# High and low value halves in one stationary for four of nine key blocks, the missing column summed by GpSimd; key copy by DMA; first expert weights split in pieces

## The reference, cut to what matters

```python
q_pool = q.reshape(B, H, S // 2, 2, D).mean(axis=3)          # [2, 8, 576, 64]
scores = scale * np.matmul(q_pool, k.transpose(0, 1, 3, 2))  # [2, 8, 576, 1152]
attn = np.exp(scores - np.max(scores, axis=-1, keepdims=True))
attn = attn / (np.sum(attn, axis=-1, keepdims=True) + 1e-09)
x = np.matmul(attn, v)                                        # [2, 8, 576, 64] -> 1152 tokens x 512
# then a mixture of 8 experts with the top two for each token (512 -> 1024 -> 512, relu),
# then h = x @ w_in [512, 2048];  out = (h * cos(h)) @ w_out
```

## Time and profile before

| | us |
|---|---|
| median of 3 runs | 854.96 |
| profiled execution: time | 854.54 |
| profiled execution: span of its instructions | 852.8 |
| TensorE matmuls busy | 838.9 |
| TensorE weight loads busy | 744.4 |
| VectorE busy | 499.0 |
| ScalarE busy | 422.2 |
| GpSimd busy | 402.5 |

### The profile page before, as it was taken

One profiled execution on the slowest core, in us unless ns is written; L12 is line 12 of the kernel. 1 busy time (PEld: TensorE's weight loads), 2 busy tenths in 40 slices (PEclk: granted clock), 3 DMA queues, 4 the chain that ended last, 5 costly groups with the idle time before them and its releaser, 6 DMA issues.

```text
span 852.8 us, 15404 instructions
## 1 busy us (share of the span) xinstructions
PE 838.9 (98%) x4868; PEld 744.4 (87%) x4869; DVE 499.0 (59%) x995; ACT 422.2 (50%) x776; POOL 402.5 (47%) x293
## 2 busy tenths in 40 slices
PE   7999999999999999999999999999999999999998
PEld 6899999999999888888887888888888888999997
DVE  7788877888877887322232222222276776676664
ACT  3777777777777763212111211111145665564554
POOL 8554445555877104648959959577532030000000
PEclk9999999999999999999999999999999999999999
DMA  5112211142232015987645545363444020000101
GB/s 146 53 43 62 64 42 42 42 142 67 92 130 102 1 56 181 310 298 241 237 151 172 197 148 184 118 214 115 155 133 152 1 75 27 12 1 0 38 1 38
DMA packets 51521, 91.28 MB, mean 107 GB/s; under 512 B 9376, under 2 KB 18592, under 8 KB 50976
## 3 DMA queue, kind: packets, MB, share of 16 engines
q1 hardware_dynamic: 40832, 67.26, 23.5%
q0 software_dynamic: 3360, 11.01, 4.4%
q10 hardware_dynamic: 7296, 12.59, 4.4%
HBM read 73.78 MB, written 17.06 MB: 107 GB/s over the span
## 4 chain that ended last, share of the span: by engine, by line
PE 89%; DVE 5%; ACT 2%; issue 2%; POOL 2%; DMA 0%; DVEq 0%; POOLq 0%; ACTq 0%
PE ps L1640 10%; PE ps L1642 10%; PE ps L1641 10%; PE ps L1460 5%; PE ps L1490 5%; PE ps L1506 4%; PE ps L1508 4%; PE ps L1507 4%; PE ps L1491 4%; PE ps L1766 4%; PE ps L1767 4%; PE ps L1765 4%; PE ps L1752 3%; PE ps L1750 3%; PE ps L1751 3%; PE ps L1679 2%
## 5 line engine op out<-in xcount | busy, mean ns | idle before, releaser
L639 POOL TENSOR_TENSOR W<-stage,W 128x2048 fp32r<-128x2048 f32 x32 | 147.3, 4602 | 2.6
L1023 DVE TENSOR_REDUCE mx<-ps 128x1 f32<-128x384 f32 x225 | 119.6, 551 | 17.8 <-PE ps L1460 17.8
L1035 DVE TENSOR_TENSOR pl__80<-ps,ph 128x576 fp32r<-128x576 f32 x144 | 108.0, 750 | 33.5 <-ACT ps L793 33.4
L788 ACT ACTIVATE ph<-ps 128x576 fp32r<-128x576 f32 x144 | 93.9, 652 | 53.5 <-PE ps L1491 52.4
L793 ACT ACTIVATE ps<-ps 128x576 f32<-128x576 f32 x144 | 93.5, 649 | 0.0
L1506 PE MATMUL ps<-ph,vs 128*65 128x288 f32 x288 | 86.1, 299 | 0.4 <-ACT ot L747 0.4
L862 ACT CAST hh<-ps 128x512 fp32r<-128x512 f32 x50 | 26.9, 590 | 119.2 <-PE ps L1679 115.2
L1490 PE MATMUL ps<-qat,kt 128*128 128x288 f32 x288 | 83.8, 306 | 1.3 <-ACT qbt L740 0.6
L1508 PE MATMUL ps<-ph,vs 128*65 128x288 f32 x288 | 84.8, 294 | 0.0
L1507 PE MATMUL ps<-pl__80,vs 128*65 128x288 f32 x288 | 84.6, 294 | 0.0
L1640 PE MATMUL ps<-W,xh 128*128 (+1 forms) x200 | 80.4, 402 | 1.3 <-POOL W L639 0.7
(11 more groups left out here) (220 smaller groups left out, 1960.8 us busy)
## 6 DMA issues: line engine op xcount, KB each, us to landing
stage<-in_moe_w_dram SPq DMA_DIRECT2D x32, 1024.0 KB
y_slots<-ys ACTq DMA_DIRECT2D x25, 256.0 KB
x_slots<-ring SPq DMA_DIRECT2D x22, 256.0 KB
xs<-x_slots ACTq DMA_DIRECT2D x22, 256.0 KB
kn<-in_k_dram SPq DMA_DIRECT2D x16, 288.0 KB, 3.3
vn<-in_v_dram SPq DMA_DIRECT2D x16, 288.0 KB, 2.8
stage<-in_moe_w_in_dram SPq DMA_DIRECT2D x4, 1024.0 KB
stage<-in_moe_w_out_dram SPq DMA_DIRECT2D x4, 1024.0 KB
```

Of the source, the lines that this page charges most:

```text
L639: pl.tensor_tensor(W[:, slot, 1, part], stage[:, j % 2, :], W[:, slot, 0, part].bitcast(F32), ALU.subtract).then_inc(w_ready, 1)
L1023: ve.tensor_reduce(mx3[:, i:i + 1], ps[:, bank_of(hh, ("m", i)), 0:PIECE], AX_X, ALU.max).then_inc(m_ev, 1)
L1035: ve.tensor_tensor(pl_[:, j % 3, :].rearrange("p (a n) -> p a n", a=2), ps[:, 2 * s_par(hh, j):2 * s_par(hh, j) + 2, 0:HQ], ph[:, j % 3, : ...
```

## The change

`SUMMED` names the key blocks 0, 2, 4 and 6. For these, and for all heads but the last, `products` uses one stationary of 128 columns: 64 high values, the ones, and the first 63 of the 64 low values. It multiplies `ph` by it in one matmul where there were two, and writes 128 partitions. `pl_` is multiplied by the 65 high columns as before. The 64th low column is left out; GpSimd multiplies `ph` of each summed block by that column (one scalar for each key, `product`), adds the four results (`add_product`), and after block 8 two matmuls with the constant stationary `e_last` add the sum over keys to row 63 of the output. `turner`, which turns the output, now adds the 63 low rows to the high ones, and so reads 128 rows.

ScalarE's exponential now waits for `one_done` before it overwrites a `ph` buffer that GpSimd reads, and TensorE waits for `sum_done` before the `e_last` matmuls. `qa` is written by a copy of `qp` instead of a second addition, and the high values by a copy.

`copy_k` moves from GpSimd to SP, as a DMA from `kt` to `k1` (64 partitions, 288 KB), issued after the keys and queries of the head two later and ahead of that head's values. Four more small gate loads fill the added rows of `turner`.

The first expert's two first pieces are loaded before the keys of head 2, the other two after the loop. GpSimd splits them in 16 chunks of 512 columns: one each with heads 2 to 9 and 12 to 15, and four after them. `lg` moves to another place, and three fills are added.

```diff
+SUMMED = (0, 2, 4, 6)
+NSUM = len(SUMMED)
+CHUNK = 512
...
@@ sync, load_head
+            def copy_k(m, par):
+                sp.wait_ge(kq_ev, 4 * (m + 1))
+                sp.dma_start(k1[0:D, par, :].bitcast(F32), kt[0:D, par, :].bitcast(F32)).then_inc(k1_in[par], 16)
...
+                if not isinstance(m, int) or m >= 2:
+                    copy_k(m - 2, par)
                 at_least(sp, v_ready, m - 1)
...
+                    sp.dma_start(turner[D + 1:P, b * H:(b + 1) * H, D + 1 + n * E:D + 1 + (n + 1) * E],
+                                 gate.rearrange("(h d) e -> d h e", d=D)[0:D - 1]).then_inc(gate_in, 16)
...
+            sp.wait_ge(kq_ready, 1)
             for j in range(2):
                 stage_piece(0, j, pieces0[j])
+            load_head(1, 0)
+            load_head(1, 1)
+            with sp.Fori(2, NHEAD // 2 - 2) as p:
+                load_head(p, 0)
+                load_head(p, 1)
+            for j in range(2):
+                sp.wait_ge(w0_done, 4 * (j + 1))
+                stage_piece(0, 2 + j, pieces0[2 + j], again=False)
@@ gpsimd
+            def product(h, par, n):
+                j = SUMMED[n]
+                pool.wait_ge(ph_done, KC * h + j + 1)
+                if n == 0:
+                    pool.wait_ge(v_ready, h + 1)
+                if n != 1:
+                    at_least(pool, sum_done, (NSUM - 1) * h + max(n - 1, 0))
+                else:
+                    at_least(pool, av_done, KC * h)
+                pl.tensor_scalar(one_sum[:, :] if n == 0 else low_sum[:, :], ph[:, j % 3, :].bitcast(F32),
+                                 vs[:, par, j, 1, D - 1:D].bitcast(F32), None, ALU.mult).then_inc(one_done, 1)
+            def add_product(h, n):
+                pool.wait_ge(one_done, NSUM * h + n + 1)
+                out_ = low_sum[:, :] if n == NSUM - 1 else one_sum[:, :]
+                pl.tensor_tensor(out_, low_sum[:, :].bitcast(F32), one_sum[:, :], ALU.add).then_inc(sum_done, 1)
...
+            def head_work(p, par, chunk, staged):
+                m = 2 * p + par
+                product(m - 2, par, 0)
+                split_q(p, par)
+                product(m - 2, par, 1)
+                add_product(m - 2, 1)
+                if chunk is not None:
+                    high_chunk(chunk, staged)
+                product(m - 2, par, 2)
+                add_product(m - 2, 2)
+                low_q(p, par)
+                if chunk is not None:
+                    low_chunk(chunk, staged)
+                product(m - 2, par, 3)
+                split_v(m - 1, 1 - par, p + par, ahead=m - 2)
@@ scalar, cycle
                         at_least(act, av_done, s - 2)
+                        h, old = 2 * p + hh - 1, (j - 3) % KC
+                        if old in SUMMED and not (j >= 3 and isinstance(h, int) and h == NHEAD - 1):
+                            at_least(act, one_done, NSUM * (h if j >= 3 else h - 1) + SUMMED.index(old) + 1)
@@ tensor, scores_t
-                    pe.wait_ge(k1_done, h + 1)
+                    pe.wait_ge(k1_in[par], 16 * (p + 1))
@@ tensor, products
+                summing = not (isinstance(h, int) and h == NHEAD - 1)
+                summed = summing and j in SUMMED
+                both = vs[:, par, j, :, :].rearrange("p t d -> p (t d)")[:, 0:P]
                 for a in range(2):
                     cols = slice(a * HQ, (a + 1) * HQ)
                     dst = ps[0:D + 1, 4 + a, 0:HQ]
-                    pe.matmul(dst, vs[:, par, j, 0, :], ph[:, j % 3, cols], start=(j == 0), stop=False)
-                    pe.matmul(dst, vs[:, par, j, 0, :], pl_[:, j % 3, cols], start=False, stop=False)
-                    last = pe.matmul(dst, vs[:, par, j, 1, :], ph[:, j % 3, cols], start=False, stop=(j == KC - 1))
+                    end = j == KC - 1 and not summing
+                    if summed:
+                        pe.matmul(ps[:, 4 + a, 0:HQ], both, ph[:, j % 3, cols], start=(j == 0), stop=False)
+                    else:
+                        pe.matmul(dst, vs[:, par, j, 0, :], ph[:, j % 3, cols], start=(j == 0), stop=False)
+                        pe.matmul(dst, vs[:, par, j, 1, :], ph[:, j % 3, cols], start=False, stop=False)
+                    last = pe.matmul(dst, vs[:, par, j, 0, :], pl_[:, j % 3, cols], start=False, stop=end)
+                if summing and j == KC - 1:
+                    pe.wait_ge(sum_done, (NSUM - 1) * (h + 1))
+                    for a in range(2):
+                        last = pe.matmul(ps[:, 4 + a, 0:HQ], e_last[:, :], low_sum[:, a * HQ:(a + 1) * HQ],
+                                         start=False, stop=True)
                 last.then_inc(av_done, 1)
```

More of the change, by code:

```diff
@@ L142, in build @@
         kq_ev = sem("kq_ev")
-        k1_done = sem("k1_done")
+        k1_in0 = sem("k1_in0")
+        k1_in1 = sem("k1_in1")
+        one_done = sem("one_done")
+        sum_done = sem("sum_done")
+        w0_high = sem("w0_high")
+        w0_done = sem("w0_done")
         m0_done = sem("m0_done")
@@ L305, in build @@
         zcol, at = place("zcol", at, [P, 1])
+        e_last, at = place("e_last", at, [P, P], F32R)
         sine, at = place("sine", at, [P, 1])
@@ L337, in build @@
         ot, at = place("ot", at, [P, QW])
+        lg, at = place("lg", at, [P, RT, 2 * E])
         assert at <= STG, (at, STG)
@@ L473, in _, with stage_piece @@
                                  gate.rearrange("(h d) e -> d h e", d=D)).then_inc(gate_in, 16)
[L474 to L480, removed]
+                    sp.dma_start(turner[D + 1:P, b * H:(b + 1) * H, D + 1 + n * E:D + 1 + (n + 1) * E],
+                                 gate.rearrange("(h d) e -> d h e", d=D)[0:D - 1]).then_inc(gate_in, 16)
+            def stage_piece(before, j, part, again=True):
+                if again:
+                    at_least(sp, w_ready, before + j - 1)
                 sp.dma_start(stage[:, j % 2, :].rearrange("p (c f) -> p c f", f=part.shape[2]), part
@@ new lines, in _ @@
+            pool.wait_ge(zeroed, FILLS - 3)
+            split_q(0, 1)
+            low_q(0, 1)
+            split_v(0, 0, 1)
+            pool.wait_ge(stage_in[0], 16)
+            pool.wait_ge(stage_in[1], 16)
+            for m in range(2, NHEAD):
+                if m == 12:
+                    pool.wait_ge(stage_in[0], 32)
+                    pool.wait_ge(stage_in[1], 32)
+                chunk = m - 2 if m < 10 else m - 4 if m >= 12 else None
+                head_work(m // 2, m % 2, chunk, chunk if m < 12 else m - 12)
@@ new lines, in _ @@
+            product(NHEAD - 2, 0, 0)
+            high_chunk(12, 4, last=True)
+            product(NHEAD - 2, 0, 1)
+            add_product(NHEAD - 2, 1)
+            low_chunk(12, 4, last=True)
+            high_chunk(13, 5, last=True)
+            product(NHEAD - 2, 0, 2)
+            add_product(NHEAD - 2, 2)
+            low_chunk(13, 5, last=True)
+            high_chunk(14, 6, last=True)
+            product(NHEAD - 2, 0, 3)
+            split_v(NHEAD - 1, 1, NHEAD // 2, ahead=NHEAD - 2)
@@ L671, in gather @@
+            low_chunk(14, 6, last=True)
+            high_chunk(15, 7, last=True)
+            low_chunk(15, 7, last=True)
             def gather(t, dst, done):
@@ L746, in o_move @@
                 at_least(act, ot_done, g)
-                sc.copy(ot[0:D + 1, 0:SQ].rearrange("p (a n) -> p a n", a=2), ps[0:D + 1, 4:6, 0:HQ]
-                        ).then_inc(ot_ev, 1)
+                rows = slice(0, D + 1 if isinstance(g, int) and g == NHEAD - 1 else P)
+                sc.copy(ot[rows, 0:SQ].rearrange("p (a n) -> p a n", a=2), ps[rows, 4:6, 0:HQ]).then_inc(ot_ev, 1)
             def soft_noise(b):
@@ L1473, in turn_o @@
                 pe.wait_ge(ot_ev, g + 1)
+                rows = slice(0, D + 1 if isinstance(g, int) and g == NHEAD - 1 else P)
                 for c in range(QC):
-                    last = pe.matmul(ps[:, bank_of(hh, ("o", 0)), c * TURN:(c + 1) * TURN], ot[0:D + 1, c * P:(c + 1) * P],
-                                     turner[:, bass.ds(g, 1), :].rearrange("p o n -> p (o n)"), start=True, stop=True)
+                    last = pe.matmul(ps[:, bank_of(hh, ("o", 0)), c * TURN:(c + 1) * TURN], ot[rows, c * P:(c + 1) * P],
+                                     turner[rows, bass.ds(g, 1), :].rearrange("p o n -> p (o n)"), start=True, stop=True)
                 last.then_inc(ot_done, 1)
```

85 lines of the change are left out of this document (43 added, 42 removed).

## The result

The changed kernel takes 886.19 us, the median of four runs (884.98 to 886.7), against 855.38 us (853.73 to 855.94) for four runs of the kernel before. The ratio is 1.0362, with a 95% interval of 1.0343 to 1.038: slower by 3.6%. I had forecast 849.8 us in a range of 843 to 857, faster. The direction is wrong, and the time lies outside the range.

The account below looks back on a forecast made before the run. TensorE was taken to bound attention, VectorE close behind, GpSimd with room. Span 852.8 + 3.4 (start) - 8.2 (15 heads) = 848.0, with 1.7 around it 849.7, stated as 849.8 us; range 843 to 857.

Parts of the forecast that it names:

- Sum 14.9: GpSimd's operations per head with a weight chunk: 14.9 us in all, against a forecast cycle of 17.6.
- the upper ends: GpSimd's list per head at the dearest prices (product 1.34, `qa` 1.559, v 1.141): 18.9 us.
- all at zero: GpSimd's new work and the new waits on it in a cycle were to cost no time.
- rival C: GpSimd becomes the bound at `kq_ready`, awaited by TensorE at step 7: 857 to 868 us, say 861; chance 0.12.
- the milder half of C: Upper end of the forecast range, 857 us, with GpSimd as the bound.
- 0.55 us a head: Attention cycle: the part of TensorE's net 0.79 us gain that gets past VectorE; 8.2 us for 15 heads.
- the 0.3 of my lower bound: Least gain per head from TensorE's shorter list, 0.3 us, if step 8 gives nothing.
- step 8: Cycle's step for key block 8, where VectorE has a `low_p` and no maxima: 0.2 of 0.26 us gained.
- Rival B: Attention cycles: VectorE keeps the gain, 0.3 us a head left, less the start's 3.4: 854 us; chance 0.12.
- +3.4: Start: head 0's key copy queues behind other loads on SP; first scores 3.4 us later, bounds 0 and 4.5.
- Rival D: Start: TensorE's clock falls in the new 4.0 us pause, about 2 us more lost: 851.8 us; chance 0.11.
- end about 1 us into the last cycle: GpSimd's last weight chunks end there, before TensorE's `w_ready` wait; first-weights changes were counted at zero.

Follow-up runs that it names:

- a_sum8: Changed kernel with GpSimd's products and additions on 8 of 576 columns, waits, matmuls, DMA and weight chunks kept: 859.18 us.
- a_warm24: Changed kernel with 24 idle matmuls in TensorE's pause at the start: 882.32 us.
- a_tt: Changed kernel with products as broadcast two-tensor multiplications on GpSimd, low queries at once, head 0's key copy first, wait for weight pieces moved to the first chunk: 853.92 us.
- a_lowq: Changed kernel with GpSimd's low queries made right after the other splits, ahead of products 1 and 2: 883.34 us.
- a_forms: Changed kernel with each head's four GpSimd products in four different forms of operation: 876.01 us.
- a_start: Changed kernel with head 0's key copy issued ahead of the two weight pieces: 881.49 us.
- b_late_w: Kernel before, with the last of the first expert's four weight pieces split in the last cycle instead of the one before: 861.93 us.
- b_maxhalf: Kernel before, with each VectorE maximum reading 192 of its 384 columns: 849.92 us.

## Why the prediction was wrong, step by step

- **GpSimd, the step that failed.** I took 0.67 us for a product and 1.34 as its upper end. Measured: 1.73. The row that decided for the low value was the select on 128 columns, 288 ns in the earlier trace rows, because it is a scalar-type operation at the cast's rate. It is another operation, and its rate says nothing about this one. The upper end, 1.34, was drawn from two-tensor rows, as if one tensor and a scalar could not cost more than two tensors. They do. With 4 x 1.06 too little for products and some 0.4 for adds and queries, "Sum 14.9" became 19.6, above even the 18.9 of the upper ends, and "all at zero" became 18.6 us in 13 cycles and 2.4 ahead of them. The place was that of rival C, the transposes behind `kq_ready`, with a loop of 19.6 instead of 18.9. I gave C 0.12 and ended the range at 857, which I called the milder half of C though it is the lowest figure of C's own 857 to 868.
- **VectorE, wrong in size.** Forecast 0.55 us a head, measured 0.15 with GpSimd out of the way, below even the 0.3 of my lower bound. In a side by side of one cycle the last maximum of a_sum8 starts 15.0 us after the pass through `turner`, against 15.1 before, and the first one 0.1 later: the stretch of the maxima is some 0.2 shorter, where I had counted 0.3. The 0.2 of step 8 didn't come. The figures were for a VectorE that follows TensorE, while the table of halved maxima shows two engines level. Rival B, at 0.12, was the truth about TensorE's part.
- **Start, right in kind, too small.** The first scores were released by the key copy's DMA, as forecast, at 24.28 instead of 21.1: +6.6 instead of +3.4. The issue came at 14.01 instead of 13.4. The rest is the rate: I used 414 GB/s from the earlier trace rows, and the windows show 367 and 219 GB/s between 16 and 24 us, with the DMA engines' share at 1.02 and 1.06, that is, full. Some of the 6.6 is chance: five runs with the changed kernel's start have their first scores at 23.2 to 24.8, three with that of the kernel before at 17.7 to 19.7, and the means are 5.3 apart.
- **Clock.** Rival D's event took place, and the pause was longer than I had priced. At the start it cost 0.7 us by a_warm24 where I had said 2, and no more can be told from single runs; that GpSimd held the first cycle back anyway would explain it, but no run shows this. The second fall, of about 1 us in the last cycle, I hadn't seen coming.
- **Last cycle, not foreseen.** I wrote that the last chunks "end about 1 us into the last cycle" and looked only at who waits for them. In fact they met VectorE's small router operations. The last cycle grew by 3.4 us: some 2.3 by these operations, an estimate from their 2.54 us and the 0.9 us of cycle for each that a_tt, a_lowq and a_forms show, and about 1 with the clock at 1.2 GHz from 327.9 to 331.3, behind TensorE's pause of 2.05.
- **Right.** The wide stationary costs nothing that these traces show: in the changed kernel its matmuls (L1609) are followed 0.13 us later, as in the earlier trace rows.
```profile
121.67 0.30 PE L1613 MATMUL ps<-pl__81,vs 128*65 128x288 f32 x1
121.81 0.30 PE L1609 MATMUL ps<-ph,vs 128*128 128x288 f32 x1
121.94 0.29 PE L1613 MATMUL ps<-pl__81,vs 128*65 128x288 f32 x1
```
The key copies of steady cycles are covered, though one takes 4.6 us in the median and not 3.3, and everything behind attention took as long as before (541.0 and 540.9).

What stays open: why the tensor-scalar form is so slow on GpSimd, what in step 8 keeps TensorE's 0.26, and what a fallen clock costs at the start.

## What to carry to other kernels

Where an operation has no row in the trace, a row of another operation on the same engine is no bound, not even an upper one. If its count times that price could fill the engine's slack, measure the operation by itself first, or look for an engine that has a row for it (here ScalarE, 0.77 us). And when work moves in time, look for the small instructions on the other engines that it will now lie beside: a multiplication of 0.2 us had become one of 4.6.

## What the runs showed of the hardware that I had not expected

- On GpSimd a tensor-scalar operation on 576 float32 columns takes 1.65 to 1.74 us, a broadcast two-tensor one 1.15, a full two-tensor one 1.32 to 1.43, a cast 0.67. On 8 columns the tensor-scalar one still takes 306 ns, the addition 201.
- TensorE's clock fell to 1.2 GHz in a pause of 6.79 us, at the end of one of 4.30 and 1.0 us behind one of 2.05. It stayed at 2.4 GHz through the waits of 0.86 and 1.36 us in steady cycles. The length of the pause alone doesn't tell: in a_start (22.17) and b_late_w (23.45) it fell for 3.4 us with no pause near it above 0.94 us, and not in the kernel before, which has the same pause.
- The start varies by itself: with an unchanged start, the kernels b_maxhalf and b_late_w had their first scores at 19.69 and 19.02 us, the one before at 17.68. A single run can't tell a start from another by less than 2 us.
- A VectorE operation on 128x40 with both inputs in SBUF, 0.20 us alone, took 4.57 us beside a GpSimd operation of 4.52, and also waited for a GpSimd cast (0.52 and 0.64 us).
